# Token mixing's second stage: transposes of x with g times V added onto them, and the second half's tasks placed between the first hidden products

## The reference

```python
# x: (4 batches, 576 rows, 512); U: (576, 32); V: (32, 576)
# w_ch1: (512, 2048); w_ch2: (2048, 512)
def _moe_ref(x, U, V, w_ch1, w_ch2):
    xt = x.transpose(0, 2, 1)
    h = xt @ U @ V
    u = x + h.transpose(0, 2, 1)
    ch = np.maximum(u @ w_ch1, 0.0) @ w_ch2
    return (u + ch).astype(np.float32)
```

## Time and profile before

| | |
|---|---|
| median of 3 runs | 1161.12 us (1160.48 to 1161.14) |
| the profiled execution | 1161.4 us |
| its span, first to last instruction | 1159.7 us |
| mean granted TensorE clock | 0.968 |
| TensorE busy | 1074.0 us (93%) |
| VectorE busy | 521.4 us (45%) |
| ScalarE busy | 468.0 us (40%) |
| GpSimd busy | 347.7 us (30%) |

### The profile page before, as it was taken

The page is one execution under the profiler, slowest core; times in us unless marked ns, Lnnn a source line. Parts: engine busy times, 40 slices in busy tenths (PEclk is TensorE's granted clock), DMA queues, the critical chain, the costliest instruction groups (busy, mean ns, idle before and its releaser), DMA issues. The chain is left out here.

```text
span 1159.7 us, 20073 instructions
## 1 busy us (share of the span) xinstructions
PE 1074.0 (93%) x7130; PEld 942.1 (81%) x7131; DVE 521.4 (45%) x1008; ACT 468.0 (40%) x886; POOL 347.7 (30%) x325
## 2 busy tenths in 40 slices
PE   6798799999989999998999998999948999999995
PEld 5566699999879999987999996999836788887784
DVE  4465445445354444535445441322176443245631
ACT  5466544434354343446344333111134433244530
POOL 4454005523412363331326422352020111211121
PEclk9899999999999999989999999999858999999998
DMA  7777115435252361434235112020157444155511
GB/s 153 177 190 181 23 30 141 121 95 124 73 138 60 111 168 49 124 100 112 64 97 139 55 38 95 30 86 32 42 181 282 130 145 142 49 187 172 183 36 35
DMA packets 110650, 127.28 MB, mean 110 GB/s; under 512 B 67213, under 2 KB 67213, under 8 KB 110544
## 3 DMA queue, kind: packets, MB, share of 16 engines
q1 hardware_dynamic: 104480, 114.54, 35.0%
q0 software_dynamic: 3520, 10.75, 2.9%
q10 hardware_dynamic: 2544, 0.59, 0.2%
HBM read 87.90 MB, written 10.22 MB: 85 GB/s over the span
## 5 line engine op out<-in xcount | busy, mean ns | idle before, releaser
L757 ACT ACTIVATE ex<-score_banks,stat 128x576 f32<-128x576 f32 x132 | 97.7, 740 | 177.8 <-DVE stat L890 177.8
L661 PE MATMUL mlp_banks<-u_hi,w_hi 128*128 128x320 f32 (+1 forms) x512 | 157.0, 307 | 4.0 <-ACT u_hi L807 4.0
L669 PE MATMUL mlp_banks<-hid_hi,w_hi 128*128 128x320 f32 (+1 forms) x512 | 158.0, 309 | 1.0 <-DVE hid_lo L939 1.0
L899 DVE SCALAR_TENSOR_TENSOR ex<-score_banks,stat,ex 128x576 f32<-128x576 f32 x132 | 107.5, 815 | 113.3 <-ACT stat L761 107.5
L466 POOL TENSOR_TENSOR w_lo<-stage,w_hi 128x1024 fp32r<-128x1024 f32 x64 | 152.9, 2388 | 4.7
L661 PE MATMUL mlp_banks<-u_hi,w_lo 128*128 128x320 f32 (+1 forms) x512 | 151.4, 296 | 0.0
L669 PE MATMUL mlp_banks<-hid_hi,w_lo 128*128 128x320 f32 (+1 forms) x512 | 151.4, 296 | 0.0
L661 PE MATMUL mlp_banks<-u_lo,w_hi 128*128 128x320 f32 (+1 forms) x512 | 151.3, 296 | 0.0
L669 PE MATMUL mlp_banks<-hid_lo,w_hi 128*128 128x320 f32 (+1 forms) x512 | 151.3, 296 | 0.0
L462 POOL CAST w_hi<-stage 128x1024 fp32r<-128x1024 f32 x64 | 66.5, 1040 | 263.5 <-PE mlp_banks L661 223.0
L890 DVE TENSOR_REDUCE stat<-score_banks 128x1 f32<-128x576 f32 x132 | 99.4, 753 | 39.5 <-PE score_banks L594 30.4
(11 more groups left out here) (229 smaller groups left out, 2001.7 us busy)
## 6 DMA issues: line engine op xcount, KB each, us to landing
stage<-in_moe_w_ch SPq DMA_DIRECT2D x64, 512.0 KB, 3.7
w_raw<-in_moe_w SPq DMA_DIRECT2D x64, 512.0 KB, 5.3
q_tiles<-q_parts SPq DMA_DIRECT2D x30, 320.0 KB, 4.1
q_tiles<-q_parts SPq DMA_DIRECT2D x60, 160.0 KB, 4.3
k_tiles<-k_parts SPq DMA_DIRECT2D x60, 144.0 KB, 3.5
raw_q<-in_q SPq DMA_DIRECT2D x32, 128.0 KB, 2.9
raw_v<-in_v SPq DMA_DIRECT2D x32, 128.0 KB, 2.8
raw_k<-in_k SPq DMA_DIRECT2D x28, 128.0 KB, 2.7
```

What stands on the lines that cost most here:

```text
L661: last = nc.tensor.matmul(bank[:, 0:w], ch1(a, g, d, c), of[:, d, cols], start=(d == 0 and n == 0), stop=(d == KC - 1 and n == 2))
L669: last = nc.tensor.matmul(bank[:, 0:w], ch2(a, g, q, c), of[:, q, 0:w], start=(q == 0 and n == 0), stop=(q == QUARTER - 1 and n == 2))
L757: nc.scalar.activation(ex_of(n), score_of(n), ACT.Exp, bias=stat[:, n % 4, 0:1], scale=-1.0).then_inc(exp_done, 1)
L899: nc.vector.scalar_tensor_tensor(out=ex_of(n), in0=score_of(n), scalar=stat[:, n % 4, 1:2], in1=ex_of(n), op0=ALU.is_le, op1=ALU.mult, acc ...
```

## The change

In a mixed task the row blocks of x are now turned by transposes (`is_transpose`), which come first and of which the first starts the bank; the product of g4 and V comes last and is added onto them. The last block is turned with its 64 rows alone. g4 has a buffer of its own. In the list of tasks the four mixed tasks of the second half stand one each behind the first four hidden tasks, so that positions 5 to 12 of a batch (counted from 0) hold hidden and mixed tasks by turns; all later tasks keep their positions. The waits are restated by a table of positions, `AT`, in place of fixed offsets.

```diff
--- before.py
+++ after.py
@@ -50,10 +50,13 @@
 def mlp_tasks():
 
     tasks = [("token_mix", 0, 0, 0)]
-    tasks += [("mixed", k, 0, c) for k in range(2) for c in range(KC)]
+    tasks += [("mixed", 0, 0, c) for c in range(KC)]
     for r in range(NQ):
         for k in range(2):
-            tasks += [("hidden", k, r, q) for q in range(QUARTER)]
+            for q in range(QUARTER):
+                tasks.append(("hidden", k, r, q))
+                if (k, r) == (0, 0):
+                    tasks.append(("mixed", 1, 0, q))
             tasks += [("channel", k, r, c) for c in range(KC)]
     tasks += [("logits", k, 0, 0) for k in range(2)]
     tasks += [("rows", 0 if i < BLOCKS[0][1] else 1, i, 0) for i in range(NT)]
@@ -65,7 +68,7 @@
 TAIL = 2 + NT
 BY_ACT = [k in ("token_mix", "mixed", "hidden", "rows") for k, *_ in TASKS]
 BY_DVE = [k in ("token_mix", "mixed", "hidden", "channel", "logits") for k, *_ in TASKS]
-GROUP0 = 1 + 2 * KC
+AT = {task: m for m, task in enumerate(TASKS)}
 PER_GROUP = 2 * (QUARTER + KC)
 
 
@@ -119,7 +122,7 @@
 
     g, i = divmod(x - RING, PIECES_G)
     b, r = divmod(g, NQ)
-    return b * NTASK + GROUP0 + r * PER_GROUP + (PER_GROUP // 2 + QUARTER - 1 if i < 2 else PER_GROUP - 1)
+    return b * NTASK + AT[("hidden" if i < 2 else "channel", 1, r, QUARTER - 1)]
 
 
 def pieces_by_step():
@@ -174,7 +177,8 @@
     least = sb("least", [P, 1])
     tau = sb("tau", [P, 6])
     ident, gates = A.ident, A.gates
-    g4 = hid_hi[:, 0:2, :].rearrange("p a b -> p (a b)")[:, 0:D]
+    g4_home = sb("g4", [P, D], F32R)
+    g4 = g4_home[:]
     v_rows = z[:, 0:S]
     first_q = u_lo[:].rearrange("p a b -> p (a b)")[:, 0:2 * PAD].rearrange("p (t n) -> p t n", t=2)
     first_k = u_hi
@@ -646,13 +650,13 @@
                 if k == 0 and c == 0:
                     pe.wait_ge(v4_made, 3)
                     pe.wait_ge(dve_task, emptied(BY_DVE, b * NTASK))
-                nc.tensor.matmul(bank[:, 0:w], g4[:, c * P:(c + 1) * P], v4[:, START[k]:START[k] + w], start=True, stop=True)
                 for n, i in enumerate(range(*BLOCKS[k])):
-                    last = nc.tensor.matmul(bank[:, n * P:n * P + ROWS[i]], x[:, i, c * P:(c + 1) * P], ident[:, 0:ROWS[i]],
-                                            start=False, stop=True, skip_group_check=True)
+                    nc.tensor.matmul(bank[:, n * P:n * P + ROWS[i]], x[0:ROWS[i], i, c * P:(c + 1) * P], ident[0:ROWS[i], 0:ROWS[i]], is_transpose=True,
+                                     start=(n == 0), stop=False, skip_group_check=True)
+                last = nc.tensor.matmul(bank[:, 0:w], g4[:, c * P:(c + 1) * P], v4[:, START[k]:START[k] + w], start=False, stop=True, skip_group_check=True)
             elif kind == "hidden":
                 if r == 0 and c == 0:
-                    pe.wait_ge(dve_task, emptied(BY_DVE, b * NTASK + KC * (k + 1)))
+                    pe.wait_ge(dve_task, emptied(BY_DVE, b * NTASK + AT["mixed", k, 0, KC - 1]))
                 if k == 0 and c == 0:
                     pe.wait_ge(w_split, PIECES_G * g + 2)
                 cols = slice(START[k], START[k] + w)
@@ -664,12 +668,12 @@
                     pe.wait_ge(w_split, PIECES_G * g + PIECES_G)
                 for q in range(QUARTER):
                     if c == 0:
-                        pe.wait_ge(dve_task, emptied(BY_DVE, t - QUARTER + q))
+                        pe.wait_ge(dve_task, emptied(BY_DVE, b * NTASK + AT["hidden", k, r, q]))
                     for n, (a, of) in enumerate(((w_hi, hid_hi), (w_hi, hid_lo), (w_lo, hid_hi))):
                         last = nc.tensor.matmul(bank[:, 0:w], ch2(a, g, q, c), of[:, q, 0:w], start=(q == 0 and n == 0), stop=(q == QUARTER - 1 and n == 2))
             elif kind == "logits":
                 pe.wait_ge(loaded_gate, 32)
-                pe.wait_ge(dve_task, emptied(BY_DVE, b * NTASK + NTASK - TAIL - 1 - (1 - k) * (QUARTER + KC)))
+                pe.wait_ge(dve_task, emptied(BY_DVE, b * NTASK + AT["channel", k, NQ - 1, KC - 1]))
                 for n, i in enumerate(range(*BLOCKS[k])):
                     for d in range(KC):
                         last = nc.tensor.matmul(bank[:, n * 16:n * 16 + E + 1], z_at(k, d, n * P, P), w_gate[:, d], start=(d == 0), stop=(d == KC - 1))
@@ -911,7 +915,7 @@
             dve.wait_ge(inv_ready, 2 * p + k + 1)
             dve.wait_ge(o_turned, 2 * p + k + 1)
             if b:
-                dve.wait_ge(task_done, (b - 1) * NTASK + 2 + k * KC + pp)
+                dve.wait_ge(task_done, (b - 1) * NTASK + AT["mixed", k, 0, pp] + 1)
             cols = slice(pp * P, (pp + 1) * P)
             last = nc.vector.tensor_tensor(x[:, 2 * k:2 * k + 2, cols].rearrange("p i (h d) -> p i h d", h=2),
                                            aux[:, 512 * k:512 * k + 2 * P].rearrange("p (i h d) -> p i h d", h=2, d=DH),
@@ -941,9 +945,9 @@
             elif kind == "channel":
                 dve.wait_ge(task_done, t + 1)
                 if r == 0:
-                    dve.wait_ge(act_task, emptied(BY_ACT, b * NTASK + KC * k + c + 1))
+                    dve.wait_ge(act_task, emptied(BY_ACT, b * NTASK + AT["mixed", k, 0, c]))
                 else:
-                    dve.wait_ge(dve_task, emptied(BY_DVE, t - PER_GROUP))
+                    dve.wait_ge(dve_task, emptied(BY_DVE, b * NTASK + AT["channel", k, r - 1, c]))
                 nc.vector.tensor_tensor(z_at(k, c, 0, w), bank[:, 0:w], z_at(k, c, 0, w), ALU.add).then_inc(dve_task, 1)
             elif kind == "logits":
                 dve.wait_ge(task_done, t + 1)
```

## The result

The changed kernel takes 1170.92 us, the median of 13 runs (1164.45 to 1178.57); the kernel before took 1163.51 us in 13 runs beside them (1160.48 to 1167.77). The ratio is 1.0064 with a 95% interval of 1.0039 to 1.0089: slower by some 7 us. The profiled execution of the changed kernel took 1173.8 us (span 1172.0), 3 us over its median; that of before, 1161.4, lies 2 us under the median of its 13 runs. So the two profiles differ by more than the kernels do, and I compare them stage by stage. The clock's part in it is no accident of the profiled execution: over the 13 executions of the changed kernel the mean granted clock has a median of 0.958 (the fastest, 1164.45 us, 0.966; the slowest, 1178.57 us, 0.952), and over 28 of the kernel before, run beside the first experiments, 0.968.

A forecast was written before the change was run, and what follows sets the result against it. TensorE is busy 93% of the span, but in mixing stages it waits for ScalarE and VectorE. Three stages at -0.28 us (-0.85) and -0.1 in the last make some -1.0 us: 1160.1 us, range 1156.8 to 1163.2.

The forecast's parts named there:

- the clock falls: Rival: transposes in steps 3 to 5 let the clock fall, 1.9 us a batch, 1167.7 us in all; chance 0.12.
- step 4: Fifth step of a pair beside attention: a mixed product shorter by 0.25 us brings the next scores from 133.90 to 133.65.
- H0: A batch's first hidden task, now right behind the last first-half mixed task; waits until ScalarE and VectorE have drained that one.
- step 5: Beside attention: H0 waits until 134.97, then runs 1.5 us; scores come at 138.00 (138.06 before), so the 0.25 is spent.
- the row at 310 us: Profile window 310 to 312 us, transposes of z after gate products: TensorE fully busy, clock 0.50; cited for the clock rival.
- The saving of a second-half task: Transposes for fp32 products in a second-half mixed task: one record of about 0.10 us less per product, 0.3 us a task.
- no saving: Lower bound for the transposes: each still takes two records; as a rival about 1161.4 us, no change, chance 0.08.
- The stage beside attention: Each of three mixing stages that run beside attention: -0.28 us, three times, so -0.85 us.
- step 6: Beside attention: third hidden task waits for the second's bank, starts at 142.07 (first hidden product 142.16 before); scores 0.09 earlier.
- The wait of the second channel task: Step 8 beside attention: it waits for the last mixed task's bank until 152.3, ending at 153.83; next scores before came at 154.11.
- the one row of 4.0 us: Profile row: first hidden product waits 4.0 us in four batches, about 1.0 each; taken to say the four stages repeat each other.
- The last stage: Mixing stage running alone: first channel product 14.8 us after first mixed against 14.95, so -0.1 us; hidden tasks 2.64 us apart.

The follow-up runs named there:

- the filling: Changed kernel with the product of g4 and V issued twice more ahead of the transposes in each first-half mixed task; 1166.24 us, 1.0031 of the kernel before.

## Why the prediction was wrong

**The step that failed is the choice between the forecast and its rival "the clock falls".** All terms of the forecast were worked out at a granted clock of 1.00, and the rival got 0.12. The evidence against it was that the stage holds 1.00 though TensorE idles 6.8 of 38 us. That row shows that the clock holds, not by how much, and the change was about to take out records in just that stage. The rival's numbers were near: 1.9 us a batch forecast, 1.7 to 1.8 measured where it fell; 1167.7 us forecast for four batches, 1170.9 measured. That is in part luck: beside attention it fell one step earlier, on the value products of step 4 and not on H0 and the turning of step 5; it fell in three stages, not four; and only 5.4 of the 12.3 us between the two profiles lie in the stages at all. The range ended at 1163.2 because it left this case out; with the stage this near to the fall it should have held it. What the runs showed in place of a held clock: mean granted clocks of 0.93, 0.93 and 0.79 in three of the four stages, 1.7 us each in the two beside attention and about 1 in the last (16.7 against 15.6 with the filling), gone when TensorE is given enough work beside the transposes.

**The reason given for the rival did not hold.** I took it, with the Trainium skill (TensorE: Matmul & The Clock Gate, PE-mode transpose), that transposes do not count for the clock. The runs with two and with three transposes per block keep 1.00 in the stages beside attention, so no run here shows that rule, and in those stages it does not hold. What the change did was to halve the turning records in a stage that had little else. Nor was the row at 310 us evidence for it. The same trace of before shows the order of things there:

```profile
308.00:310.00 2.00, 2.00 (x19) 2.00 (x19) 0.00 (x0) 1.20 (x3) 0.00 (x0) 0.94 0.00 0
...
307.47 3.04 PE L675 MATMUL mlp_banks<-w_gate,z 128*128 128x9 f32 x24
310.37 1.95 PE L679 MATMUL mlp_banks<-ident,z 128*128 128x128 f32 x8
```

The clock falls at 309.8 us, during the gate products; the first transpose of z starts at 310.37. In the last stage a fall came with the order alone too, all products kept, at a place where the kernel before does the same and keeps its clock.

**The saving of a second-half task was mis-sized.** A first-half task came out as priced at 0.2 us (from its first record to the next instruction 0.56 us before, 125.40 to 125.96, and 0.35 after, 327.58 to 327.93). For a second-half task I priced the transpose by attention's, at 0.10 us a record, and the last block has 64 rows: its three transposes take 0.51 us, not 0.3. The task saved under 0.1 us in place of 0.3. The rows of before had no 64-row transpose, and the bound "no saving" was there but not used for this one.

**The stage beside attention: -0.28 forecast; +0.1 measured with the clock held** (186.4 against 186.3, the first stage), so the sign was wrong. The 0.25 in step 4 came: the scores of step 5 start 14.74 us after token mixing, before 15.01. It was spent in steps 5 and 6 as forecast, and 0.3 more: step 6's stalled hidden product starts at 144.84, 23.5 us after token mixing, forecast 23.2. The wait of the second channel task is there as worked out: first channel product to the next scores 4.12 us, before 3.54. So the sum of the moved waits was right within 0.4 us a stage. That the four stages repeat each other doesn't follow from the one row of 4.0 us, as I had it (it is 1.14 three times and 0.61); the equal intervals of 25.2 us show it for the three beside attention.

**The last stage.** The 2.64 us between hidden tasks was 2.70. With the clock held (the filled kernel) 4.9 + 10.7 = 15.6 us where 14.8 was forecast; its first part contains the filling. As the change stands, with its fall, it is 16.7.

**That nothing changes for the other queues, the splits and the stores** shows in the stage times: from the scores behind the second channel task to the gate products both kernels take 151.1 us in the first batch (154.11 to 305.19 before, 156.62 to 307.72 after).

**Open.** Some 3 us of the difference between the two kernels' profiles lies between gate products and token mixing, where the code is the same (38.8 us in both profiles of the changed kernel, 35.2 and 35.7 in both of before). The clock falls there in every profile, at times that shift with what went before. The falls inside the mixing stages don't explain it: the six kernels that kept 1.00 in all four stages, other than the kernel before, took 36.4 to 38.6 us there (the one with two full transposes per block, which fell in the last, 35.5). Whether the changes make it fall longer or it is chance isn't told apart by single profiles. The start of the kernel, too, differs between profiles by over 4 us (first token mixing at 117.3 to 121.6 us) before any changed instruction runs.

## What to carry to other kernels

Where a stage waits for other engines, work taken off TensorE brought nothing here, and it cost: the granted clock fell, and the 20 value products that ran then took 4.07 us in place of 2.38. Before such a cut ask not whether the clock holds in that stage but how much work would be left in it. And putting a short task between two long ones that share two buffers trades one engine's waiting for another's: work out when each buffer comes free.

## What the runs showed of the hardware

- Adding TensorE work shortened a stage: with two more products per first-half task 25.0 us in place of 26.3 beside attention, 15.6 in place of 16.7 alone, with the granted clock at 1.00 in place of 0.93 and 0.79.
- A transpose of a 64-row block among full ones took about 0.35 us, a full one 0.09: the weight loads stand 0.17 us before its own starts. Turning 64 rows of zeros as well cost less than leaving them out.
- The clock fell to 1.2 GHz both where TensorE was fully busy by its records (products of 9 columns, 2.00 of 2.00 us at 308 to 310) and where it waited half of the time (2.1 of 4.0 us busy ahead of the value products). The same code kept 1.00 in the changed kernel's first stage and fell in the next two. Busy time by the records does not tell which.
- What a fall cost depended on what ran in it: 1.7 us on the value products, nothing among the last mixed tasks of a stage that waits for other engines (186.2 us from token mixing to the gate products, 186.3 without a fall).
